# Two queues for the first loads, one warm-up tensor from VectorE, and weight loads set between others, in a linear-attention kernel with two feed-forward layers

## What is computed

```python
# attention: 4 sequences, 8 heads, 768 steps, 64 columns a head
gamma = 1.0 - 2.0 ** (-5.0 - np.arange(H))
for t in range(S):
    state = gamma * state + k[:, :, t] (outer) v[:, :, t]
    y[:, :, t] = q[:, :, t] @ state / sqrt(D)
x = y as 3072 tokens x 512
# first layer, d_ff 2048
h = x @ w_in;  g = where(h > 0, h, exp(min(h, 0)) - 1);  x = g @ w_out
# second layer, d_ff 1024
h = x @ w_in2; solu = h * softmax(h); ln = layer norm of solu * g_ln; out = ln @ w_out2
```

## Time and profile before

| | |
|---|---|
| median of 3 runs | 842.25 us (841.95 to 843.55) |
| the profiled execution | 846.07 us, of which the span 844.2 us |
| TensorE matmul | 835.6 us busy, 99% of the span |
| TensorE weight loads | 692.9 us, 82% |
| VectorE, ScalarE, GpSimd | 65%, 49%, 47% |
| granted clock, DMA | full; 87 GB/s over the span, near 400 GB/s in the first tenth |

### The profile page before, as it was taken

How to read it: one execution, slowest core, us unless ns; L and a number is a source line. 1 busy time by engine, 2 the same in 40 slices (tenths; PEclk the granted TensorE clock), 3 DMA queues, 4 the chain that set the end, 5 groups by cost and what they waited for, 6 DMA issues and landing times.

```text
span 844.2 us, 12588 instructions
## 1 busy us (share of the span) xinstructions
PE 835.6 (99%) x4850; PEld 692.9 (82%) x4850; DVE 551.4 (65%) x850; ACT 416.8 (49%) x671; POOL 392.7 (47%) x448
## 2 busy tenths in 40 slices
PE   8999989999999999999999999999999999999998
PEld 6998878888888888888888888888888888888886
DVE  4687666768635555575355455788977777777773
ACT  3686656565535555554455555563333433334422
POOL 3688675754016575620257661564443334344200
PEclk9999999999999999999999999999999999999999
DMA  9999500105003010140201001612111111111001
GB/s 341 394 392 335 193 26 26 50 26 178 1 0 100 26 50 25 31 169 1 74 26 50 26 26 62 188 50 76 50 50 50 51 50 51 39 51 50 25 14 50
DMA packets 49071, 73.31 MB, mean 87 GB/s; under 512 B 2930, under 2 KB 23666, under 8 KB 48756
## 3 DMA queue, kind: packets, MB, share of 16 engines
q1 hardware_dynamic: 48864, 72.43, 25.2%
q10 hardware_dynamic: 148, 0.08, 0.0%
HBM read 55.72 MB, written 16.78 MB: 86 GB/s over the span
## 4 chain that ended last, share of the span: by engine, by line
PE 88%; DVE 4%; DMA 3%; SPq 2%; ACT 1%; issue 1%; POOL 1%; DVEq 0%; ACTq 0%; POOLq 0%
PE ps L686 10%; PE ps L682 10%; PE ps L683 10%; PE ps L635 8%; PE ps L637 8%; PE ps L636 8%; PE ps L694 4%; PE ps L795 4%; PE ps L797 4%; PE ps L796 4%; PE ps L696 4%; PE ps L695 4%; PE ps L576 2%; PE ps L781 2%; PE ps L604 2%; DMA k<-units_dram 1%
## 5 line engine op out<-in xcount | busy, mean ns | idle before, releaser
L492 POOL TENSOR_TENSOR u_lo<-u_raw,u_hi 128x256 fp32r<-128x256 f32 x168 | 142.4, 881 | 191.6 <-ACT u_hi L1166 191.6
L683 PE MATMUL ps<-g_hi,wd_lo 128*128 128x512 f32 x384 | 149.4, 389 | 0.0
L682 PE MATMUL ps<-g_hi,wd_hi 128*128 128x512 f32 x384 | 149.4, 389 | 0.0
L686 PE MATMUL ps<-g_lo,wd_hi 128*128 128x512 f32 x384 | 149.4, 389 | 0.0
L635 PE MATMUL ps<-x_hi,u_hi 128*128 128x512 f32 x336 | 132.0, 393 | 2.3 <-ACT p L1231 2.3
L636 PE MATMUL ps<-x_hi,u_lo 128*128 128x512 f32 x336 | 131.4, 391 | 0.0
L637 PE MATMUL ps<-x_lo,u_hi 128*128 128x512 f32 x336 | 131.3, 391 | 0.0
L487 POOL TENSOR_TENSOR u_raw<-u_raw 128x256 f32<-128x256 f32 x96 | 89.0, 927 | 19.3 <-DMA u_raw<-w_dram 13.3
L683 PEld LDWEIGHTS ps<-g_hi,wd_lo 128*128 128x128 f32 x384 | 72.1, 188 | 15.1
L686 PEld LDWEIGHTS ps<-g_lo,wd_hi 128*128 128x128 f32 x384 | 72.1, 188 | 15.0
L682 PEld LDWEIGHTS ps<-g_hi,wd_hi 128*128 128x128 f32 x384 | 72.1, 188 | 14.8
(11 more groups left out here) (94 smaller groups left out, 1488.1 us busy)
## 6 DMA issues: line engine op xcount, KB each, us to landing
u_raw<-w_dram SPq DMA_DIRECT2D x24, 512.0 KB, 3.5
q<-units_dram SPq DMA_DIRECT2D x12, 512.0 KB, 7.4
k<-units_dram SPq DMA_DIRECT2D x12, 512.0 KB, 9.0
v<-units_dram SPq DMA_DIRECT2D x12, 512.0 KB, 8.2
x_between<-x SPq DMA_DIRECT2D x24, 256.0 KB, 2.7
x_raw<-x_between SPq DMA_DIRECT2D x12, 512.0 KB, 3.5
out_dram<-y_sb SPq DMA_DIRECT2D x24, 256.0 KB, 2.0
kn<-units_dram SPq DMA_DIRECT2D x10, 512.0 KB, 10.0
```

Of the source, the lines that this page charges most:

```text
L492: nc.gpsimd.tensor_tensor(u_lo[n % 2][:, o, :], u_raw[n % 2][:, o, :], u_hi[n % 2][:, o, :].bitcast(f32), ALU.subtract).then_inc(ul_done, 1)
L682: nc.tensor.matmul(ps[:, bank + m, :], hi, g_hi[:, no % 3, :], start=(f == 0), stop=False)
L683: nc.tensor.matmul(ps[:, bank + m, :], lo, g_hi[:, no % 3, :], start=False, stop=False)
L686: last = nc.tensor.matmul(ps[:, bank + m, :], hi, g_lo[:, no % 3, :], start=False, stop=(f == NF1 - 1))
```

## The change

Four things. Loads of k and kn for steps 0 to 2 go to ScalarE's queue, ahead of its own work; SyncE keeps their q and v, in the order q, v. `warm` is zeroed by VectorE, and there are 8 products instead of 4 ahead of L729. GpSimd decays q in two instructions, each with its own count, and `scores` waits for each half by itself. In the loop VectorE does one sum of x in each of steps 4 to 7 and `split_x_lo` 0 to 2 in steps 8 to 10, so 3 to 6 come behind it; and SyncE issues wd(2) to wd(5) ahead of the first layer's u loads, and wd(6) to wd(15) two at a time behind u(2) to u(6).

```diff
-WARM = (4, 4)
+WARM = (8, 4)
...
-                load(s, q_sb, 0, q_in)
-                if s < EARLY:
-                    load(s, k_sb, 1, k_in)
-                    load(s, v_sb, 3, v_in)
-                else:
-                    load(s, v_sb, 3, v_in)
-                    load(s, k_sb, 1, k_in)
-                if s % NC < NC - 1:
-                    load(s, kn_sb, 2, kn_in)
+                load(sp, s, q_sb, 0, q_in)
+                load(sp, s, v_sb, 3, v_in)
+                if s >= SLOTS:
+                    load(sp, s, k_sb, 1, k_in)
+                    if s % NC < NC - 1:
+                        load(sp, s, kn_sb, 2, kn_in)
...
-            for f in range(2, NF1):
+            for f in range(2, 6):
                 load_wd(f)
...
+                    if blk == 0 and i < NFP - 3:
+                        load_wd(2 * i + 6)
+                        load_wd(2 * i + 7)
...
-            nc.gpsimd.memset(warm[:, :], 0.0).then_inc(warm_zeroed, 1)
...
-                q = q_sb[s % SLOTS]
-                nc.gpsimd.tensor_tensor(q, q, q_decay[:, :].unsqueeze(1).to_broadcast([P, 2, HH * C]), ALU.mult)\
-                    .then_inc(q_decayed, 1)
+                for one in range(2):
+                    q = q_sb[s % SLOTS][:, one, :]
+                    nc.gpsimd.tensor_tensor(q, q, q_decay[:, :], ALU.mult).then_inc(q_decayed, 1)
...
-                if s >= EARLY:
-                    pe.wait_ge(q_decayed, s - EARLY + 1)
                 for one in range(2):
                     if s < EARLY:
                         pe.wait_ge(q_early, 2 * s + one + 1)
+                    else:
+                        pe.wait_ge(q_decayed, 2 * (s - EARLY) + one + 1)
...
+            nc.vector.memset(warm[:, :], 0.0).then_inc(warm_zeroed, 1)
...
-                for i in {4: (0,), 5: (1, 2), 6: (3,)}.get(s, ()):
-                    sum_x(0, i)
-                if 7 <= s < 11:
-                    split_x_lo(0, s - 7)
-            for i in range(4, 7):
+                if 4 <= s < 8:
+                    sum_x(0, s - 4)
+                elif 8 <= s < 11:
+                    split_x_lo(0, s - 8)
+            for i in range(3, 7):
                 split_x_lo(0, i)
...
             act.dma_start(q_rows[0:2, :], q_table).then_inc(q_rows_in, 16)
-            act.dma_start(decays[:, :], tables[:, T_DECAYS:T_DECAYS + C + 2 * H]).then_inc(decays_in, 16)
+            for s in range(SLOTS):
+                load(act, s, k_sb, 1, k_in)
+                if s == 0:
+                    act.dma_start(decays[:, :], tables[:, T_DECAYS:T_DECAYS + C + 2 * H]).then_inc(decays_in, 16)
+                load(act, s, kn_sb, 2, kn_in)
```

More of the change, by code:

```diff
@@ L315, in raw_ready, with load @@
                     engine.wait_ge(w3_in[k], 16)
+        def load(queue, s, to, i, done):
+            n, _ = step_chunks(s)
+            queue.dma_start(to[s % SLOTS], units[n:n + NC + 1:NC, :, 512 * i:512 * (i + 1)].rearrange("t p c -> p t c"))\
+                .then_inc(done[s % SLOTS], 16)
         block = ctx.enter_context(nc.Block())
@@ L320, in _ @@
         def _(sp):
[L321 to L324, removed]
             def load_step(s):
```

## The result

The changed kernel takes 844.76 us (median of 18 runs, 843.59 to 845.62), the kernel before 842.93 in 18 runs beside it (841.48 to 845.54). The ratio is 1.0020, interval 1.0013 to 1.0027: slower by 1.8 us, just clear of the scatter. 840.0 was forecast, with 838.2 to 842.4 as the range, and 0.10 for slower.

The account below looks back on a forecast made before the run. TensorE was taken as the bound, its matmuls busy 99% of the span. -3.0 us at the first layer's start and +0.8 from two queues gave -2.2, off the median of 842.25: 840.0 us, range 838.2 to 842.4.

Parts of the forecast that it names:

- the low clock behind the wait: ... 1.73 us: Behind M2 of pair 2's wait: twelve matmuls, 4.45 us at the low clock, would take 2.72, saving 1.73 us.
- the sum of -3.0: First layer's start: moved wd loads and VectorE's new order together remove a 1.27 us wait and 1.73 us of low clock.
- I take the difference off the median of 842.25: Whole kernel: the -2.2 us is subtracted from the timed median, though the profiled execution lay 3.8 us above it.
- the 1.15 that VectorE takes back: M7 of pair 0: VectorE's fourth low part behind the loop delays U2, so TensorE loses 1.15 us.
- the 1.24 to 1.76 that set the bounds: VectorE's added low part: 1.24 us uncontended or 1.76 slowed by GpSimd, giving a loss of 0.9 to 1.4 us.
- "+0.8 us" by v of step 2: Start, two queues: v of step 2 lands one or two places later, delaying step 2's `key_values`; +0.8 us.
- The warm-up and the halves, costed at nothing: Start: 8 first products costed at 0; GpSimd's q decay in two instructions, nothing behind step 2.
- neither decides, because `key_values` of step 0 needs v: Step 0: scores done by 11.4 or near 9 don't matter, since v landed at 8.8 and wants 1.28 us of ScalarE.
- +0.7 at most: Step 0: upper limit in us of the longer warm-up's cost, otherwise taken as 0.
- the lateness of the next part: Start: the two queues' delay, +0.8 us, was seen as covering any cost of the longer warm-up.
- Rival 2: Start: v of step 2 last or ScalarE held issuing, +1.7, 840.9 us; with low clock 842.7. Chance 0.22.
- Rival 4: Start: two interleaved queues move less, at 319 GB/s; v of step 2 late, sum +3.6, 845.8 us. Chance 0.08.

Follow-up runs that it names:

- experiment 2: Only the wd loads moved (SyncE issues ten of fourteen behind u(2)), against the kernel before: 840.54 us, ratio 0.9972.
- 4: Wd loads moved and VectorE's sums and low parts in the new order, against the kernel before: 841.86 us, ratio 0.9993.
- 3: Only VectorE's sums and low parts put in the new order, against the kernel before: 842.42 us, ratio 0.9993.
- 5: Only the loads of steps 0 to 2 split over two queues, against the kernel before: 844.42 us, ratio 1.0015.
- 7: Loads of steps 0 to 2 in two queues, added to the kernel with only the wd loads moved: 843.25 us, ratio 1.0002 to the kernel before.
- 6: Only the two queues, with the small decays table issued ahead of k of step 0, against the kernel before: 845.44 us, ratio 1.0033.
- 8: Wd loads moved; first twelve loads in one queue, in the two queues' landing order: 841.38 us, ratio 0.9988 to the kernel before.
- 15: The changed kernel with the loads of steps 0 to 2 back in one queue, old order: 843.30 us, ratio 1.0010 to the kernel before.
- 1: The kernel before, unedited, timed and profiled a second time: 842.4 us, ratio 0.9993.
- 16: The changed kernel with VectorE's sums and low parts in the old order: 843.63 us, ratio 1.0015 to the kernel before.
- 12: Wd loads moved and 2 instead of 4 products between the small product and the first scores: 840.33 us, ratio 0.9978 to the kernel before.

## Why the prediction was wrong

**The stage behind attention: mechanism right, size wrong.** The step that failed is the term "the low clock behind the wait: ... 1.73 us" in the sum of -3.0 and, with it, "I take the difference off the median of 842.25". The stall was real in each trace of the kernel before, and moving the wd loads took it away as worked out (the copy's wait gone, `u_hi` with almost no idle time). But only 27 executions of 142 show a stretch at the low clock, and the profiled one was among them. I had the sign of it before me: that execution lay 3.8 us above the median. I subtracted its difference from a median of executions that mostly didn't have it. Moving the wd loads is worth 2.3 us (experiment 2), the stall alone, and not the 4.1 that the prediction comes to for it (3.0 and the 1.15 that VectorE takes back).

**VectorE's added low part: right, a little small.** Forecast 1.15 us on M7 of pair 0 (0.9 to 1.4); 1.05 us lost there in the trace of 4, and 1.3 by the time. In the changed kernel M6's 0.32 us comes on top, which no term had, and the added low part takes 2.0 us there (6.62 for four, 4.59 for three), outside the 1.24 to 1.76 that set the bounds. It was also right that the two go together: alone it costs nothing (3), since the stall takes it up. So "-3.0 us" for the pair should have been -1.0 by these two; 4 against the kernel before gives 0.9993.

**The two queues: "+0.8 us" by v of step 2.** Direction right, the wait and the size wrong: this is the second step that failed. 1.6 us alone (5) and 2.7 on top of edit 2 (7). I had q and k of a step land together, then v and kn, and then followed v only. In the changed kernel's trace v of every step came sooner than before. k of step 0 and kn of steps 0 and 1, the loads in ScalarE's queue, came later, and they start `scores` and `key_values` with no work between to take the delay up. Experiments 6 to 8 show that the table isn't the cause, that the order alone is a third to a half, and that the rest comes with a load of each queue moving at the same time: the two queues are served alike, as the prediction took it, but SP's queue is two loads ahead, so v is paired with kn of the step before, and both loads of a pair are as late as the second. Why the first of ScalarE's loads lands anywhere from 7.5 to 9.6 us is open.

**The warm-up and the halves, costed at nothing.** Medians say 0.8 to 0.9 and 0.4, each measured twice, none of them outside its interval. The working for the warm-up ("neither decides, because `key_values` of step 0 needs v") held in the execution with the early clock, where that wait was 1.3 us. With the late clock the scores are done 1.6 us later than that. The "+0.7 at most" was near. The prediction covered it by the lateness of the next part; that part came elsewhere, so nothing covered it.

Added up on the ruler of experiment 2: 2.7 + 1.3 + 0.8 + 0.4 - 2.3 = +2.9, against the measured +1.8. They don't simply add: the longer warm-up and the late k of step 0 delay the same scores, which would fit the 0.8 that 15 gives the queues in the changed kernel. That is argued, not shown.

The traces, one of each kernel, give the same account by stages, in us:

| | to step 2's scores | from there to the first layer | from there to the end | span |
|---|---|---|---|---|
| before, as predicted from | 20.6 | 55.6 | 768.0 | 844.2 |
| before, again (1) | 19.3 | 56.2 | 765.9 | 841.4 |
| edit 2 alone | 19.6 | 55.6 | 763.4 | 838.6 |
| the changed kernel | 22.1 | 56.1 | 765.3 | 843.5 |

Against the second trace of the kernel before, the start loses 2.8 us where +0.8 was forecast, and what lies behind attention gains 0.6 where -3.0 was forecast: 2.5 from the stall, less the 1.9 that VectorE's order takes there. The first trace was late at the start and had the low clock behind the stall, and taking it as typical made the change look better both times.

Of the rivals, none is what happened. Rival 2 had the extra 1.7 us at the start, but by a late v and with -3.0 beside it; its low clock behind an idle start does show, in the trace of 16. Rival 4 put the slower case on a lower rate, and the rate was 404 GB/s between 8.5 and 20.6 us.

The best kernels are 2 and 12, 840.5 and 840.3: the moved wd loads, in 12 with two products fewer, 0.28% and 0.22% faster than the kernel before.

## What to carry to other kernels

Before a stall is priced from a trace, see where that execution stands among the timed ones: a clock that falls behind the stall belongs to some executions only, and its share goes into the sum with that chance. When loads are dealt to a second queue, list for each load who waits for it with no slack, those that go to the second queue first: here the bandwidth was the same, but the loads landed in pairs, the first as late as the second. And price a change together with the stall that it may hide in: an edit that costs nothing alone (3) cost 1.3 us once its neighbour had removed the stall (4).

## What the runs showed that I had not expected

A wait of 2.3 us before M2 of pair 2 was the same in two traces, and in one of them TensorE fell to the lower clock behind it and in the other it didn't; over 142 executions a low mean clock shows in 19%, at 2.1 us each. Two queues moved bytes at the rate of one, but landed them in pairs 2.5 us apart instead of singly 1.3 us apart, so that the same load came up to 1.6 us later. And 8 warm-up products raised the clock by 6 us in three of five traces and not before 8.5 in the other two, with the same start; with 4 it was never up before the scores.
